# One level of Strassen's form in the first layer of a dense mixture, on one Trainium2 core

## The reference

```python
def _moe2_ref(x, domain_probs, w1, w2):      # x 1152x512, w1 4x512x1024, w2 4x1024x512
    p = domain_probs / (domain_probs.sum(-1, keepdims=True) + 1e-09)
    out = np.zeros((N, D), dtype=np.float32)
    for e in range(E):
        h = np.maximum(x @ w1[e], 0.0)       # first layer
        out += p[:, e:e + 1] * (h @ w2[e])   # second layer
    return out
```

## Time and profile before

| | us |
|---|---|
| median of 3 runs | 672.31 (670.12 to 673.67) |
| profiled execution, its own time | 669.75 |
| its span, first to last instruction | 667.7 |
| dense mixture, first to last matmul | 261.04 to 658.63 |
| mean granted TensorE clock | 0.984 |
| PE busy / PEld / DVE / ACT / POOL | 630.0 / 553.1 / 250.5 / 166.7 / 177.1 |

### The profile page before, as it was taken

How to read it: one execution, slowest core, us unless ns; L and a number is a source line. 1 busy time by engine, 2 the same in 40 slices (tenths; PEclk the granted TensorE clock), 3 DMA queues, 4 the chain that set the end, 5 groups by cost and what they waited for, 6 DMA issues and landing times.

```text
span 667.7 us, 9552 instructions
## 1 busy us (share of the span) xinstructions
PE 630.0 (94%) x3449; PEld 553.1 (83%) x3450; DVE 250.5 (38%) x483; ACT 166.7 (25%) x405; POOL 177.1 (27%) x128
## 2 busy tenths in 40 slices
PE   5979678999999999999999999999999999999994
PEld 4869566678876788999999999999999999999993
DVE  5777647752258423222222222222222222222221
ACT  4766316742257322111111111111111111111110
POOL 7433272006200000343503503404404404300111
PEclk9989798999999999999999999999999999999998
DMA  9906047883225000030210300300300400100111
GB/s 239 214 18 251 34 173 242 284 294 94 79 92 192 31 16 16 2 114 13 79 49 0 97 31 0 102 26 0 121 5 0 125 0 0 63 0 0 47 47 47
DMA packets 24878, 54.01 MB, mean 81 GB/s; under 512 B 5912, under 2 KB 8600, under 8 KB 24856
## 3 DMA queue, kind: packets, MB, share of 16 engines
q1 hardware_dynamic: 16904, 28.78, 14.0%
q0 software_dynamic: 6080, 21.52, 9.6%
q10 hardware_dynamic: 1872, 3.41, 1.8%
HBM read 48.70 MB, written 5.00 MB: 80 GB/s over the span
## 4 chain that ended last, share of the span: by engine, by line
PE 82%; DVE 4%; POOL 3%; issue 3%; DMA 3%; SPq 3%; ACT 1%; DVEq 0%; ACTq 0%; POOLq 0%
PE bank L1058 30%; PE bank L1070 29%; PE bank L1012 8%; PE bank L1024 7%; POOL x_by_rank L396 2%; PE bank L996 1%; DVE w_lo L773 1%; DMA x_tile<-x_by_rank 1%; SPq L284 1%; PE bank L890 1%; PE bank L911 1%; PE bank L943 1%; DVE w_lo L779 1%; DMA dprob<-in_moe_domain_probs 1%; PE bank L990 1%
## 5 line engine op out<-in xcount | busy, mean ns | idle before, releaser
L549 ACT ACTIVATE h_hi<-bank 128x384 fp32r<-128x384 f32 x92 | 45.3, 492 | 335.3 <-PE bank L1058 335.3
L1058 PE MATMUL bank<-x2T_hi,u_hi 128*128 128x384 f32 x384 | 128.6, 335 | 0.0
L1058 PE MATMUL bank<-x2T_hi,u_lo 128*128 128x384 f32 x384 | 128.6, 335 | 0.0
L1058 PE MATMUL bank<-x2T_lo,u_hi 128*128 128x384 f32 x384 | 128.4, 334 | 0.0
L414 POOL CAST u_hi<-u_raw 128x2048 fp32r<-128x2048 f32 x16 | 30.3, 1892 | 313.5 <-PE bank L1070 267.4
L1070 PE MATMUL bank<-u_hi,h_lo 128*128 128x512 f32 x288 | 112.5, 391 | 0.0
L1070 PE MATMUL bank<-u_lo,h_hi 128*128 128x512 f32 x288 | 112.5, 390 | 0.0
L1070 PE MATMUL bank<-u_hi,h_hi 128*128 128x512 f32 x288 | 112.0, 389 | 0.0
L832 DVE SCALAR_TENSOR_TENSOR h_lo<-bank,h_hi 128x384 fp32r<-128x384 f32 x96 | 53.5, 557 | 153.1 <-ACT h_hi L549 147.2
L843 DVE SCALAR_TENSOR_TENSOR acc<-bank,meta_s,acc 128x512 f32<-128x512 f32 x63 | 44.2, 750 | 122.1 <-PE bank L1070 122.1
L416 POOL TENSOR_TENSOR u_lo<-u_raw,u_hi 128x2048 fp32r<-128x2048 f32 x16 | 73.9, 4616 | 1.3
(11 more groups left out here) (169 smaller groups left out, 730.2 us busy)
## 6 DMA issues: line engine op xcount, KB each, us to landing
w_raw<-in_moe_w SPq DMA_DIRECT2D x10, 2048.0 KB, 8.6
u_raw<-in_moe_w POOLq DMA_DIRECT2D x16, 1024.0 KB, 5.5
x_tile<-x_by_rank ACTq DMA_DIRECT2D x13, 256.0 KB, 2.7
qT<-in_qT SPq DMA_DIRECT2D x4, 576.0 KB, 8.1
kT<-in_kT SPq DMA_DIRECT2D x8, 288.0 KB, 9.9
v_rows<-in_v_by_position SPq DMA_DIRECT2D x12, 128.0 KB, 10.4
v_rows<-in_v_by_residue SPq DMA_DIRECT2D x8, 126.0 KB
x_by_rank<-zero_row SPq DMA_DIRECT2D x1, 256.0 KB, 2.8
```

What stands on the lines that cost most here:

```text
L549: a.activation(h_hi[:, f, :], bank[f][:, 0:SB], ACT.Relu).then_inc(g_hi_kept, 1)
L1058: last = t_.matmul(bank[f][:, 0:SB], lhs[half][:, c, cols], rhs[:, c, tok], start=n == 1, stop=n == 3 * DC)
```

## The change

The first layer x @ w1[e] is seen as a product of 2x2 blocks: x is split in two halves of tokens (0 to 575 and 576 to 1151) and two of inner values (chunks 0, 1 and 2, 3), w1 in two of inner values and two of hidden units. Strassen's form (Winograd's variant) takes seven block products for eight. In w1's blocks A11, A12, A21, A22 the sums are S1 = A21 + A22, S2 = S1 - A11, S3 = A11 - A21, S4 = A12 - S2, and four differences T of x's blocks stand beside them. P1 to P7 are written `product(n, s, page, k)`.

The work is cut into 16 steps (four experts, four slices f) of 256 hidden units, 128 out of each half. The tokens of each half are cut in two subs s of 288. A product is six matmuls of 288 columns (two chunks, three parts), and a step has 14 of them, 84 matmuls, then nine output tiles z of six matmuls of 512 columns, 54. Products 1, 6, 7 and 4 run up one sum in bank s; in between ACT copies the sum to part (U: P1, P1+P6, P1+P6+P7). DVE makes the three other blocks of h in pre (c11 = P1 + P2, c22 = third U + P5, c12 = second U + P5 + P3). ACT takes the relu of each (keep_hi), DVE the rest (keep_h_lo). z alternates between banks 5 and 6.

Once, at the start, the x blocks are summed from hi and lo (sum_x; sub 0 on DVE, sub 1 on POOL), T made in place on DVE (make_t), and both cut again (cut_t on ACT, split_t on DVE). POOL makes S1 to S4 per step and cuts seven blocks of u1 and 256 rows of u2; loads are now three for u1 (rows of 512 bytes) and one for u2 per step, 1 MB together. The copy to y_tile moves from DVE to ACT. First loads of both weights are issued together, after the fourth y_tile.

```diff
+            def load_u1(n):
+                e, f = divmod(n, FS)
+                for i, slots in ((0, ((0, DC, 1),)), (1, ((0, KC, 0), (KC, DC, 3)))):
...
+            def split_u1(n):
+                pool.wait_ge(u1_in, 48 * (n + 1))
+                a21, a11, a12, a22 = (u1_raw[:, k] for k in range(4))
+                s1, s2, s3, s4 = (u1_raw[:, k] for k in range(4, 8))
+                g.tensor_tensor(s1, a21, a22, ALU.add).then_inc(u_summed, 1)
+                g.tensor_tensor(s3, a11, a21, ALU.subtract).then_inc(u_summed, 1)
...
+                g.tensor_tensor(s2, s1, a11, ALU.subtract).then_inc(u_summed, 1)
...
+                g.tensor_tensor(s4, a12, s2, ALU.subtract).then_inc(u_summed, 1)
...
+                g.tensor_copy(u1_hi[n % 2][:], u1_raw[:, 1:8]).then_inc(u1_hi_cut, 1)
...
+                g.tensor_tensor(u1_lo[n % 2][:], u1_raw[:, 1:8], u1_hi[n % 2][:].bitcast(FP32), ALU.subtract)\
...
# ACT, the order of a step (s is the second argument)
+            def keep_step(n):
+                keep_part(n, 0, 0)
+                keep_hi(n, 0, 0, 0)
+                keep_part(n, 0, 1)
+                keep_part(n, 1, 0)
+                keep_part(n, 0, 2)
+                keep_hi(n, 1, 0, 0)
+                keep_hi(n, 0, 1, 1)
+                keep_part(n, 1, 1)
+                keep_hi(n, 0, 1, 0)
+                keep_hi(n, 0, 0, 1)
+                keep_part(n, 1, 2)
+                keep_hi(n, 1, 1, 1)
+                keep_hi(n, 1, 1, 0)
+                keep_hi(n, 1, 0, 1)
# DVE
+            def make_c12(n, s):
+                dve.wait_ge(c_done[s], n * 2 + 2)
+                w.tensor_tensor(pre[s][2][:], bank[2 + s][:, 0:SUB], part[s][1][:], ALU.add).then_inc(pre_made[s], 1)
...
+            step(sum_x(0, 0))
+            step(sum_x(0, 1))
+            make_t(0, 0, 0)
+            make_t(0, 1, 0)
+            make_t(0, 1, 1)
+            make_t(0, 0, 1)
...
+            split_t(0, 0, 0)
+            split_t(0, 1, 0)
+            keep_lo(n_tiles, at_end, x2_whole)
+            split_t(0, 1, 1)
+            split_t(0, 0, 1)
...
+            keep_h_lo(0, 0, 0, 1)
+            dve.wait_ge(x_summed, 2)
+            make_t(1, 0, 0)
+            make_t(1, 1, 0)
+            make_t(1, 1, 1)
+            make_t(1, 0, 1)
+            split_t(1, 0, 0)
+            split_t(1, 1, 0)
+            split_t(1, 1, 1)
+            split_t(1, 0, 1)
+            first_z(0)
+            first_z(1)
+            first_z(2)
+            make_c22(0, 1)
...
+            def keep_step(n, e, f):
+                make_c11(n, 0)
+                keep_h_lo(n, 0, 0, 0)
+                make_c11(n, 1)
+                make_c22(n, 0)
+                keep_h_lo(n, 1, 0, 0)
+                keep_h_lo(n, 0, 1, 1)
+                keep_h_lo(n, 0, 1, 0)
+                make_c12(n, 0)
+                keep_h_lo(n, 0, 0, 1)
+                make_c22(n, 1)
+                keep_h_lo(n, 1, 1, 1)
+                keep_h_lo(n, 1, 1, 0)
+                add_z(n, e, f, 0)
+                make_c12(n, 1)
+                keep_h_lo(n, 1, 0, 1)
+                for i in range(1, NT):
+                    add_z(n, e, f, i)
# PE
+                if k in (6, 7, 4):
+                    pe.wait_ge(part_kept[s], n * 3 + {6: 1, 7: 2, 4: 3}[k])
+                if k == 3:
+                    pe.wait_ge(pre_made[s], n * 3 + 2)
...
+            def h_u2(n, f, i, page, at_start=False):
+                t, at = Z_ORDER[i], Z_BANK[(NT * f + i) % 2]
+                if i == 0:
+                    pe.wait_ge(u2_split, n + 1)
+                    pe.wait_ge(h_lo_kept[0], n * 4 + 4)
+                if i == sum(is_first_sub(t) for t in range(NT)):
+                    pe.wait_ge(h_lo_kept[1], n * 4 + 4)
+                if not at_start or i > 1:
+                    pe.wait_ge(z_added, n * NT + (i - 1))
...
+            product(0, 0, 0, 1)
+            product(0, 0, 0, 2)
             flip_y(n_tiles)
+            product(0, 1, 0, 1)
+            pe.wait_ge(xt_kept, n_tiles + 1)
+            product(0, 1, 0, 2)
+            pe.wait_ge(t_split[0], 1)
+            product(0, 0, 0, 5)
+            pe.wait_ge(t_split[0], 4)
+            for k in (6, 7, 4, 3):
+                product(0, 0, 0, k)
+            h_u2(0, 0, 0, 0, True)
+            pe.wait_ge(x2_whole, 1)
+            h_u2(0, 0, 1, 0, True)
+            h_u2(0, 0, 2, 0)
+            pe.wait_ge(t_split[1], 4)
+            for k in (5, 6, 7, 4, 3):
+                product(0, 1, 0, k)
+            for i in range(3, NT):
+                h_u2(0, 0, i, 0)
+
+            def whole_step(n, f):
+                page = f % 2
+                for s, k in ((0, 1), (0, 2), (0, 5), (0, 6), (1, 1), (1, 2), (0, 7), (1, 5), (1, 6), (0, 4), (0, 3), (1, 7)):
+                    product(n, s, page, k)
+                h_u2(n, f, 0, page)
+                product(n, 1, page, 4)
+                product(n, 1, page, 3)
+                for i in range(1, NT):
+                    h_u2(n, f, i, page)
```

More of the change, by code:

```diff
@@ L545, in _ @@
                             cut_w1(c)
[L546 to L549, removed]
-            at_end = act.value_load(tile_at[0:1, bass.ds(n_tiles, 1)], min_val=0, max_val=N)
-            act.wait_ge(g_done, 1)
-            a.activation(h_hi[:, 0, :], bank[0][:, 0:SB], ACT.Relu).then_inc(g_hi_kept, 1)
+                    act.wait_ge(y_done, j + 1)
@@ L555, in _ @@
             act.wait_ge(xt_in, n_tiles * 16 + 16)
[L556 to L560, removed]
+            keep_hi(0, 0, 0, 0)
+            keep_part(0, 1, 0)
+            keep_part(0, 0, 1)
+            keep_part(0, 0, 2)
+            keep_hi(0, 1, 0, 0)
+            keep_hi(0, 0, 1, 1)
@@ L862, in _ @@
[L862 to L865, removed]
+            make_c11(0, 0)
+            keep_h_lo(0, 0, 0, 0)
+            make_c11(0, 1)
+            make_c22(0, 0)
+            keep_h_lo(0, 1, 0, 0)
+            keep_h_lo(0, 0, 1, 1)
+            keep_h_lo(0, 0, 1, 0)
+            make_c12(0, 0)
+            keep_h_lo(0, 0, 0, 1)
+            dve.wait_ge(x_summed, 2)
+            make_t(1, 0, 0)
@@ L866, in _ @@
+            for f in range(1, FS):
+                keep_step(f, 0, f)
             with dve.Fori(1, E2) as e:
[L867 to L870, removed]
+                for f in range(FS):
+                    keep_step(e * FS + f, e, f)
         @block.tensor
@@ L1062, in h_u2 @@
-            def h_u2(e, half, s):
-                hs = NSB * half + s
-                blk0 = e * (NHALF * NSB)
-                for f in range(FH):
-                    pe.wait_ge(g_lo_kept, blk0 * FH + (FH * hs + f + 1))
-                    for tt in range(SBT):
-                        ts = slice(P * tt, P * (tt + 1))
-                        for i, (lhs, rhs) in enumerate(((h_hi, u2_hi), (h_hi, u2_lo), (h_lo, u2_hi))):
-                            last = t_.matmul(bank[5 + tt][:], lhs[:, f, ts], rhs[half][:, f, :],
-                                             start=f == 0 and i == 0, stop=f == FH - 1 and i == 2)
-                        if f == FH - 1:
-                            last.then_inc(z_done, 1)
@@ new lines, in h_u2 @@
+            def h_u2(n, f, i, page, at_start=False):
+                t, at = Z_ORDER[i], Z_BANK[(NT * f + i) % 2]
+                if i == 0:
+                    pe.wait_ge(u2_split, n + 1)
[4 more added lines that the diff above has]
+                    pe.wait_ge(z_added, n * NT + (i - 1))
+                ts = slice(P * t, P * (t + 1))
+                for c in range(2):
+                    for k, (lhs, rhs) in enumerate(((h_hi, u2_hi), (h_hi, u2_lo), (h_lo, u2_hi))):
+                        last = t_.matmul(bank[at][:], lhs[:, c, ts], rhs[page][:, c, :],
+                                         start=c == 0 and k == 0, stop=c == 1 and k == 2)
+                last.then_inc(z_done, 1)
```

312 lines of the change are left out of this document (205 added, 107 removed).

## The result

| | before | after |
|---|---|---|
| median on the same chip, us | 672.78 (670.12 to 673.67, 4 runs) | 701.08 (697.35 to 702.74, 4 runs) |
| ratio to before | | 1.042 [1.0367, 1.0472] |
| profiled execution and its span, us | 669.75, 667.7 | 697.35, 695.3 |
| dense mixture, first matmul to end of the last | 397.6 | 426.1 |
| behind the last matmul, to the end of the span | 9.1 | 6.8 |

The kernel became 28.3 us slower where 16 were forecast. The sign and the places were right. The time lies 1.1 us above the upper end of the range.

What follows compares the result with a forecast made beforehand. PE's matmuls were taken to bound the kernel. First step 36.9 + 15 x 24.88 = 410.1, plus clock 3.0 and seams 1.6, made 414.7 against 397.6; less 1.15, +16.0 on 672.3 gave 688.3 us, range 677 to 700.

Steps and rivals of the forecast that it cites:

- The pace of 288 columns: On PE in the products: one matmul of 288 columns takes 0.1333 us, with bounds 0.120 and 0.1733.
- the 20.5 us saved: PE's matmuls in the dense mixture: sixteen steps take 375.0 us against 395.5, before any wait.
- z0 for h_lo: Steady step: the first z tile waits for sub 0's last h_lo, with one product as cover, and starts 1.01 us late.
- z3 for acc: Steady step: z3 uses z1's bank, needs add_z(1), which DVE reaches late, and starts 0.44 us late.
- P7 and P4 of the first step: First step: without another product between running sums, each waits 0.78 to 0.84 us for ACT's copy.
- The end: Behind the last matmul: tiles finish 1.36 us apart, so the last scatter issues 1.25 behind instead of 2.4; 1.15 saved.
- the price of DVE's operations: DVE on 288 columns takes 0.455 us, from 0.56 at 384 and 0.69 at 512; make_t takes 0.75 each.
- Cost nothing: POOL's sums and cuts, some 15 us in a step of 24.9, were to add no time.
- z2's wait: First step: z2 waits 3.53 us for first_z(0), behind eight DVE operations for sub 1.
- The clock: Behind z2's wait in the first step: about 6 us at half clock cost 3.0 us, bounds 0 and 3.5.
- the bounds: Own case: shorter hand-overs without exposed load give mixture 403.5, total 682; operations as long as at 384 columns 425.9, total 704.
- the second rival: Products on PE: a 288-column matmul takes 0.120 us, step 24.0, mixture 396.5 + 4.6, total 674.7; chance 0.08.

Runs made afterwards that it cites:

- all_three: Changed kernel with c11, c22, c12 in PSUM, products reordered, POOL held back and first_z(0) earlier in the first step: 663.44 us, ratio 0.986 to the kernel before.
- psum_start: Changed kernel with c11, c22, c12 in PSUM, POOL held until split_t is done and first_z(0) ahead of split_t: 685.39 us, one run.
- pe_order: Changed kernel with products, ACT copies and DVE operations reordered, so three products of sub 1 precede z0: 676.44 us, one run.

## Why the prediction was right in sign and too low

**Right.** The pace of 288 columns (0.1327 for 0.1333), and so the 20.5 us saved: 1.5 blocks of before took 24.82, a step without waits takes 23.53, and 16 x 1.3 = 20.6. Where PE waits and for whom: z0 for h_lo at 1.08 (1.01), z3 for acc at 0.38 (0.44) in the two steps in which POOL makes no sum, 0.75 to 0.80 at P7 and P4 of the first step (0.78 to 0.84). The step without that disturbance, 24.9, is the forecast one. The end: 2.2 saved, forecast 1.15, a small miss.

**The step that failed** is the price of DVE's operations: "DVE takes 0.56 for 384 and 0.69 for 512, so 0.455", and "the four make_t of 576 elements 0.75 each". Both rows of the first have a PSUM bank as one input. The price holds for that case (457 ns), and for two SBUF inputs while POOL reads nothing; it was applied to 96 h_lo, to make_t and to split_t, which have two SBUF inputs while POOL is busy, and there they took 700 and 1,050 ns. With it fails POOL's "Cost nothing": I asked whether POOL would be late with the weights, which it never was, and not what it does to others while it works. In the steady steps this was worth 13 x 0.35 = 4.6 us; with the second input in PSUM all steps take 24.87, 0.1 below the forecast. In the first step the waits came out 5.0 us above the forecast; by luck z2's wait, 1.5 shorter than forecast, hides a part of what P5, P6 and z0 lost.

**The clock** was a second mis-sized term: 5.0 us for 3.0, and also tied to the wrong event. I laid it to z2's wait of 3.53. It fell at 268.8, at the end of P5's wait, in which PE stood still for 3.00, and stayed down for 13.7 us and not 6; in all_three it fell behind waits of 0.67 and 1.88.

**The sums.** They come out as written, but the mixtures beside the bounds (403.5, 425.9) and the second rival (396.5, 399.1) stand without the 4.6 us of clock and seams, which the times next to them contain.

The parts, in the spans' terms:

| | forecast | measured | miss |
|---|---|---|---|
| ahead of the mixture | 0 | +1.3 | 1.3 |
| first step | 40.0 | 46.9 | 6.9 (waits 5.0, clock 2.0) |
| fifteen later steps and the last end | 374.7 | 379.2 | 4.5 |
| behind the last matmul | -1.15 | -2.2 | -1.1 |

Together this is 11.6, against 27.6 - 16.0. The +1.3 can't be laid to the change: the copy of y_tile moved to ACT, but the start of the routed mixture was already 1.6 late in that execution, under unchanged code at a lower clock.

**Where the gain of seven products for eight went:** against the 20.6 us of PE time saved stand 26 in fifteen later steps, at up to 1.8 us of waits each, and 23 in the first step over one of 23.5. all_three has no waits left in the later steps and spends 15 at the start.

**Open.** What sets when the granted clock falls isn't settled: with P5's wait cut from 3.3 to 0.9 it fell anyway in psum_start, for as long, and in all_three for half as long, though the two have the same first step. In pe_order, whose first step is that of the changed kernel, it was down for 20.5 us and not for 13.7 and 3.4. No run kept PE without a wait at the start, so that this was not tried.

## What to carry to other kernels

Price an operation by where its operands lie and by what the other engines do at that time: one price for a PSUM input, another for two SBUF inputs beside a busy GpSimd. An engine that is never late can still cost time. Where a chain of hand-overs of some 1.8 us leads to the next matmul, count the independent matmuls between, and reorder the products before anything else: that alone was worth 23 us here (one run), four times what the shorter DVE operations gave. And when a wait is cut, read who stands behind it in the program's order: z2 took back nearly all that z0 had gained.

## What the runs showed of the hardware that was not expected

- A DVE operation of 0.46 us with two SBUF inputs took up to 3.94 beside a GpSimd subtraction of 4.01, at most 1.06 with that subtraction in pieces, and 0.46 beside fills or with one input in PSUM.
- A DVE cast of 9 elements with one input, in SBUF, took 0.69 us at 274.32 beside a GpSimd sum and 0.17 in psum_start with none beside it. So not only operations with two SBUF inputs are held; no run took this apart.
- The granted clock fell to half for 13.7 us (20.5 in three other kernels) from the end of a wait of 3.0 us, and for 6.8 and 13.7 us behind waits of 0.67 and 1.88 us, while before it had been down for 3.4 and 6.8 us behind idle stretches of 4.07 and 3 us.
- GpSimd took 0.73 us for a sum of 256 elements, where the earlier trace rows in proportion give 0.58. A sum of 1152 took 2.62, as they do give, and 3.05 to 3.23 when it started beside a DVE operation with two SBUF inputs.
